# Attention probabilities scaled in place before the transpose, half blocks of two heads transposed together, half tile's values on 64 queries

## What is computed

```python
for e in range(4):
    q, k, v = x @ wq[e], x @ wk[e], x @ wv[e]
    scores = 64 ** -0.5 * (q @ k.T)                # then a causal mask
    a = exp(scores - max); a /= a.sum(-1) + 1e-9
    out += w_e * (a @ v @ wo[e])                   # w_e: gate of a token, 0 outside its best 2 experts
```

## Time and profile before

| | |
|---|---|
| median of 3 runs | 814.02 us (814.00 to 814.14) |
| the profiled execution's own time | 816.52 us |
| its span, first to last instruction | 814.4 us |
| granted TensorE clock, mean | 0.998 |
| TensorE busy | 798.5 us (98%) |
| VectorE busy | 489.7 us (60%) |
| ScalarE busy | 371.3 us (46%) |
| GpSimd busy | 186.3 us (23%) |

### The profile page before, as it was taken

The page is one execution under the profiler, slowest core; times in us unless marked ns, Lnnn a source line. Parts: engine busy times, 40 slices in busy tenths (PEclk is TensorE's granted clock), DMA queues, the critical chain, the costliest instruction groups (busy, mean ns, idle before and its releaser), DMA issues. The chain is left out here.

```text
span 814.4 us, 16834 instructions
## 1 busy us (share of the span) xinstructions
PE 798.5 (98%) x6605; PEld 720.0 (88%) x6605; DVE 489.7 (60%) x1293; ACT 371.3 (46%) x845; POOL 186.3 (23%) x239
## 2 busy tenths in 40 slices
PE   6999999999999999999999999999999999999998
PEld 5888989989899898989889898998989989898896
DVE  3878654675447855487444865468554675547740
ACT  2767423663345533556134752356323653355521
POOL 1641332013310233002330123301331013300220
PEclk9999999999999999999999999999999999999999
DMA  9956023030231205040050401404023000100001
GB/s 258 255 129 164 2 45 86 11 109 1 52 73 51 68 1 117 15 118 1 1 111 14 119 1 37 94 2 118 1 50 75 2 2 1 59 14 2 1 2 64
DMA packets 117405, 47.28 MB, mean 58 GB/s; under 512 B 94352, under 2 KB 110736, under 8 KB 117328
## 3 DMA queue, kind: packets, MB, share of 16 engines
q1 hardware_dynamic: 117328, 46.21, 22.6%
HBM read 35.19 MB, written 9.44 MB: 55 GB/s over the span
## 5 line engine op out<-in xcount | busy, mean ns | idle before, releaser
L1070 PE MATMUL w<-wsgT_s,big 128*128 128x288 f32 x768 | 107.6, 296 | 0.0
L1070 PE MATMUL t<-big,wqk_s 128*128 128x288 f32 x768 | 106.0, 296 | 1.0 <-DVE wsgT_s L950 0.9
L1070 PEld LDWEIGHTS w<-wsgT_s,big 128*128 128x128 f32 x768 | 104.0, 189 | 0.0
L1070 PEld LDWEIGHTS t<-big,wqk_s 128*128 128x128 f32 x768 | 102.5, 188 | 1.6 <-DVE wsgT_s L950 1.1
L1070 PE MATMUL w<-wout_s,big 128*128 128x512 f32 x396 | 99.1, 399 | 0.0
L610 POOL TENSOR_TENSOR yT<-squares,yT 128x256 fp32r<-128x256 f32 (+1 forms) x32 | 22.4, 699 | 316.8 <-ACT yT L740 316.8
L844 DVE CUSTOM_DVE_ANT_0 w<-w,causal 128x64 f32<-128x64 f32 (+4 forms) x160 | 75.3, 515 | 24.2 <-PE w L1101 23.1
L1070 PEld LDWEIGHTS w<-wout_s,big 128*128 128x128 f32 x396 | 72.9, 188 | 17.2 <-DVE big L887 1.6
L754 ACT ACTIVATE big<-work 128x576 fp32r<-128x576 f32 x32 | 21.9, 686 | 113.5 <-POOL work L633 94.3
L1070 PE MATMUL t<-w_s,yT 128*128 128x512 f32 x240 | 63.3, 404 | 0.0
L956 DVE TENSOR_REDUCE ss<-squares 128x8 f32<-128x512 f32 (+1 forms) x40 | 25.2, 630 | 62.6 <-ACT squares L690 62.5
(11 more groups left out here) (140 smaller groups left out, 1439.3 us busy)
## 6 DMA issues: line engine op xcount, KB each, us to landing
kin<-in_k_dram SPq DMA_DIRECT2D x8, 1024.0 KB, 6.2
vin<-in_v_dram SPq DMA_DIRECT2D x8, 1024.0 KB, 9.2
out_dram<-work SPq DMA_DIRECT2D x32, 256.0 KB, 2.1
qin<-in_q_dram SPq DMA_DIRECT2D x112, 72.0 KB, 2.4
staged_win<-in_moe_w_in_dram SPq DMA_DIRECT2D x4, 512.0 KB, 5.4
vin<-in_moe_w_sg_dram SPq DMA_DIRECT2D x4, 288.0 KB, 3.9
kin<-in_k_dram SPq DMA_DIRECT2D x8, 128.0 KB, 2.9
vin<-in_v_dram SPq DMA_DIRECT2D x8, 128.0 KB, 7.0
```

Source lines behind the costliest of these rows:

```text
L1070: last = nc.tensor.matmul(o, stationary(hs, c), mv(hm, c), start=c == of[0] and p == 0, stop=c == of[-1] and p == len(PASSES) - 1)
```

## The change

The gate and the inverse row sum are multiplied into a [128, 1] factor, and the probabilities themselves are multiplied by it in place before they are transposed: for the even n of a tile by ScalarE, for the odd n by VectorE. The padding columns of `probs` are thus free, and the layout is turned around: the keys of e = 0 are stored in reversed block order and end where those of e = 1 begin, so that the half block of 64 keys of e = 0 and that of e = 1 lie side by side and form one block of 128. A tile has 4t + 2 blocks in place of 4t + 4. The value tile of the first keys is arranged to match. `y_mul` goes; ScalarE and VectorE take the high and low parts of y from PSUM, and GpSimd has no part in it. Tile 0's weighted values are computed for its 64 real queries only.

```diff
-    T_UNITS = {t: [4] * (t + 1) if t < NT - 1 else [8, 8, 4] for t in range(NT)}
+    T_UNITS = {t: [4] * t + [2] if t < NT - 1 else [8, 8, 2] for t in range(NT)}
+    SCALE_GROUPS = [(0, 1), (2, 3), (4,), (5,), (6,), (7,), (8, 9)]
...
-        return [("pv", 2 * t), ("pv", 2 * t + 1), ("y_mul", t), ("yhi", t)]
+        return [("pv", 2 * t), ("pv", 2 * t + 1), ("yhi", t)]
...
-            plan += [("ranks", 0), ("g_exp", 0), ("weights", 0), ("qk", (0, 1)), ("scale", 0), ("qk", (EP, 1)), ("scale", 1),
+            plan += [("ranks", 0), ("g_exp", 0), ("weights", 0), ("qk", (0, 1)), ("scale", 0), ("scale", 1), ("qk", (EP, 1)),
                      ("qk", (1, 1))]
...
-        plan += [("scale", 2)] + values(0) if last else values(0) + [("scale", 2)] + KV
-        plan += [("s", 6), ("s", 7), ("T", 2), ("exp", 6)] + copies(2, 0) + [("exp", 7)] + copies(2, 1, 2) + [("scale", 3)] + values(1)
+        plan += [("scale", 2), ("scale", 3)] + values(0) + ([] if last else KV)
+        plan += [("s", 6), ("s", 7), ("T", 2), ("exp", 6)] + copies(2, 0) + [("exp", 7), ("scale", 4)] + copies(2, 1, 2) + [("scale", 5)] + values(1)
...
-    MLP = [("h", 0), ("weights", 1), ("scale", NT - 1), ("h", 1), ("gelu", 0), ("gelu", 1)] + values(3)
+    MLP = [("h", 0), ("weights", 1), ("scale", 6), ("h", 1), ("gelu", 0), ("gelu", 1)] + values(3)
...
+        def qk_bounds(m, h):
+            return (0, 320, S)[h:h + 2] if m == EP else (0, HALF, S)[h:h + 2]
+        def qk_pieces(m, h):
+            lo, hi = qk_bounds(m, h)
+            if m != EP:
+                return [(0, hi - lo, PAD + lo)]
+            return [(max(0, k0 - lo), k0 + w - lo, SP - k0 - w) for k0, w in [(0, PAD)] + [(PAD + P * b, P) for b in range(4)]
+                    if lo <= k0 < hi]
...
-                        nc.scalar.activation(vals[PAD:P, j, :], src(U)[PAD:P, 0:VW], ACT.Copy).then_inc(v_half, 1)
+                        x = src(U)
+                        nc.scalar.activation(vals[0:PAD, 0, 0:2 * HD], x[0:PAD, 0:2 * HD], ACT.Copy)
+                        nc.scalar.activation(vals[PAD:P, 0, 2 * HD:VW], x[PAD:P, 2 * HD:VW], ACT.Copy).then_inc(v_half, 1)
...
+                    elif kind == "scale":
+                        n = SCALE_GROUPS[j][0]
+                        if n % 2 == 0:
+                            act.wait_ge(scl_ready, count(part, len(SCALE_GROUPS), j + 1))
+                            for a in range(2):
+                                nc.scalar.activation(probs_of(n, a), probs_of(n, a), ACT.Copy,
+                                                     scale=row_inv[:, n, a:a + 1]).then_inc(scaled["act"], 1)
...
-                    nc.vector.tensor_tensor(
-                        probs[t % 2][:, :, :, 0:PAD].rearrange("p e a n -> p (e a) n"),
-                        invs.rearrange("p e (a d) -> p (e a) d", d=1).to_broadcast([P, E, PAD]),
-                        gate[:, t, :].rearrange("p (f d) -> p f d", d=1).to_broadcast([P, E, PAD]),
-                        ALU.mult).then_inc(row_scaled, 1)
+                    nc.vector.tensor_tensor(invs, invs, gates, ALU.mult).then_inc(scl_ready, 1)
+                    n = ns[-1]
+                    if n % 2 == 1:
+                        dve.wait_ge(scl_ready, count(part, len(SCALE_GROUPS), g + 1))
+                        for a in range(2):
+                            nc.vector.tensor_scalar(probs_of(n, a), probs_of(n, a), row_inv[:, n, a:a + 1], None,
+                                                    ALU.mult).then_inc(scaled["dve"], 1)
...
-                def y_scaled(t):
...
                 def y_low(t):
+                    o = PAD if t == 0 and part % 2 else 0
+                    x = ps[u.slot(part, ("y", t))][:, 0:2 * P].rearrange("p (e n) -> p e n", e=EP)
                     dve.wait_ge(yT_hi, count(part, NT, t + 1))
+                    give(nc.vector.tensor_tensor(yT[:, LO, :, P * t + o:P * (t + 1)], x[:, :, o:P],
+                                                 as_f32(yT[:, HI, :, P * t + o:P * (t + 1)]), ALU.subtract), ("y", t))
...
-                    pe.wait_ge(row_scaled, count(part, NT, t + 1))
-                    blocks = [(e, a, b) for e in range(EP) for a in range(2) for b in range(t + 1)]
+                    blocks = [(0, a, b) for a in range(2) for b in range(1, t + 1)] + [(None, a, 0) for a in range(2)]
+                    blocks += [(1, a, b) for a in range(2) for b in range(1, t + 1)]
...
+                            if (i, r) == (0, 0):
+                                wait_scaled(2 * t)
+                            if (e, a) == (None, 0):
+                                wait_scaled(2 * t + 1)
...
+                    real = PAD if t == 0 else 0
...
-                            last = nc.tensor.matmul(x[HD * a:HD * (a + 1), P * e:P * (e + 1)], vals[:, b, w:w + HD],
-                                                    turned(t, e, a, b), start=b == 0, stop=b == t,
+                            last = nc.tensor.matmul(x[HD * a:HD * (a + 1), P * e + real:P * (e + 1)], vals[:, b, w:w + HD],
+                                                    turned(t, e, a, b)[:, real:P], start=b == 0, stop=b == t,
                                                     skip_group_check=True)
```

More of the change, by code:

```diff
@@ L276, in moe_chain @@
         x_tile = [work[:, 512 * r:512 * (r + 1)] for r in range(2)]
-        sq_tile = sb("squares", [P, 512], F32)[:, :]
-        y_t = [sq_tile[:, 2 * P * r:2 * P * (r + 1)] for r in range(2)]
-        probs = [probs_0, staged[:, :].rearrange("p (e a n) -> p e a n", e=EP, a=2)]
+        sq_tile = staged[:, 0:512]
+        probs = [x.rearrange("p (a n) -> p a n", a=2) for x in (probs_0[:, :], staged[:, :])]
         pT = [work, qT_uT[:, :, :].rearrange("p c n -> p (c n)")]
@@ L702, in body @@
                         m, h = j
-                        nc.scalar.activation(big2[:, HI, m, PAD + HALF * h:PAD + HALF * (h + 1)], src(U)[:, 0:HALF],
-                                             ACT.Copy, scale=HD ** -0.5 if m < EP else 1.0).then_inc(qk_hi, 1)
+                        x = src(U)
+                        for lo, hi, o in qk_pieces(m, h):
+                            last = nc.scalar.activation(big2[:, HI, m, o:o + hi - lo], x[:, lo:hi],
+                                                        ACT.Copy, scale=HD ** -0.5 if m < EP else 1.0)
+                        last.then_inc(qk_hi, 1)
                     elif kind == "g_exp":
@@ L843, in maximum, with scale_rows @@
                     x = ps[slot][:, o:o + K]
-                    nc.vector.tensor_tensor_reduce(x, x, causal[:, SP - K:SP], -1.0, -MASKED, ALU.add, ALU.min,
+                    t = n // 2
+                    m0 = SP - P if t > 0 and n % 2 == 0 else SP - K
+                    nc.vector.tensor_tensor_reduce(x, x, causal[:, m0:m0 + K], -1.0, -MASKED, ALU.add, ALU.min,
                                                    neg_max[:, n, a:a + 1]).then_inc(max_ready, 1)
-                def scale_rows(t):
-                    for n in (2 * t, 2 * t + 1):
+                def scale_rows(g):
+                    ns = SCALE_GROUPS[g]
+                    for n in ns:
@@ L974, in body @@
                         if part == 0:
-                            nc.vector.memset(vals[0:PAD, 0, :], 0.0)
-                        give(nc.vector.tensor_tensor(vals[PAD:P, 0, :], ps[u.slot(part, U)][0:PAD, 0:VW], vals[PAD:P, 0, :],
+                            nc.vector.memset(vals[PAD:P, 0, 0:2 * HD], 0.0)
+                            nc.vector.memset(vals[0:PAD, 0, 2 * HD:VW], 0.0)
+                        x = ps[u.slot(part, U)]
+                        nc.vector.tensor_tensor(vals[0:PAD, 0, 0:2 * HD], x[PAD:P, 0:2 * HD], vals[0:PAD, 0, 0:2 * HD], ALU.add)
+                        give(nc.vector.tensor_tensor(vals[PAD:P, 0, 2 * HD:VW], x[0:PAD, 2 * HD:VW], vals[PAD:P, 0, 2 * HD:VW],
                                                      ALU.add), U)
@@ L983, in body @@
                         m, h = j
-                        cols = slice(PAD + HALF * h, PAD + HALF * (h + 1))
                         dve.wait_ge(qk_hi, count(part, 8, QK_NTH[j] + 1))
-                        give(nc.vector.scalar_tensor_tensor(
-                            out=big2[:, LO, m, cols], in0=ps[u.slot(part, U)][:, 0:HALF],
-                            scalar=HD ** -0.5 if m < EP else 1.0, in1=as_f32(big2[:, HI, m, cols]),
-                            op0=ALU.mult, op1=ALU.subtract), U)
+                        for lo, hi, o in qk_pieces(m, h):
+                            last = nc.vector.scalar_tensor_tensor(
+                                out=big2[:, LO, m, o:o + hi - lo], in0=ps[u.slot(part, U)][:, lo:hi],
+                                scalar=HD ** -0.5 if m < EP else 1.0, in1=as_f32(big2[:, HI, m, o:o + hi - lo]),
+                                op0=ALU.mult, op1=ALU.subtract)
+                        give(last, U)
                     elif kind == "s":
@@ L1091, in scores @@
                     V, slot, o, K = scores_at(n, 0)
```

(8 more changed lines are left out.)

94 lines of the change are left out of this document (38 added, 56 removed).

## The result

The changed kernel took 817.19 us (median of 7 runs, 815.24 to 821.24) against 814.12 us for the kernel before (7 runs, 814.00 to 814.68): ratio 1.0037, 95% interval 1.0021 to 1.0052. Measured once more beside later experiments it took 820.66 us (6 runs) against 815.94: 1.0051 (1.0032 to 1.0070). So it is slower, by 0.2 to 0.7%. The time lies inside the forecast range (808 to 819), but the forecast took no change for the likeliest (814.5) and measured is 3.1 us more. The forecast kept 817 to 821 for another cause, dearer scalings, which did not come true: that the number lies inside the range is in part luck.

What follows compares the result with a forecast made beforehand. TensorE bounds the kernel, with the ScalarE/VectorE softmax chain close behind, taking back its 1.34 us a batch. 8 x 0.1 + 8 x 0.05 - 0.3 = +0.9, taken as +0.5 on 814.02: 814.5 us, range 808 to 819.

Steps and rivals of the forecast that it cites:

- dearer scalings: Rival: ScalarE's scaling of the last two pairs and everything queued behind it take longer, 817 to 821 us; chance 0.26.
- Steps 1 to 5: Fifth batch's softmax chain: first maxima of tiles 2, 3, 4 at 449.65, 454.2, 460.0, last pair's at 463.86.
- step 3: Tile 3's exponentials end at 458.05; TensorE arrives 0.9 us earlier for tile 4's scores and waits 0.1 to 0.2 us.
- Step 6: After tile 4's exponentials: ScalarE scalings, table load, gelus, y's high part to 471.25; VectorE's copy of tile 4 ends 472.85.
- Step 7: Tile 4's weighted values start at 472.9, before 472.81: chain +0.1 us a batch where TensorE alone gives -1.34.
- The drain behind a table load: Ahead of the first gelu: the skill's rule of about 1.38 us on top, 11 us more in all; chance 0.01.
- The fall of the clock at the new wait: Rival: half clock behind the wait of about 1 us near tile 4's values, each batch: 13 us, 827; chance 0.04.
- The last batch: No k.v product fills in; the 2.04 us wait and half clock stay, two transposes less: -0.3 us.
- The step that failed: Scaling tiles 0 and 1 ahead of the second key copy: up to 0.2 us a batch without cover, counted as 0.
- that cover: Gaps hiding the key and value copies before tile 1's transposes; the early scalings eat about 0.6 us of them.
- the factor 8: Per-batch terms read in the fifth batch, taken for all eight: 8 x 0.1 + 8 x 0.05 - 0.3.
- The clock rival: Clock falling at the new wait near tile 4's values, once a batch: 13 us more, 827 us; chance 0.04.

Runs made afterwards that it cites:

- e9: Changed kernel, in the first batch alone the scalings of tiles 0 and 1 moved behind the second key copy and `wsgR`: 815.90 us, 0.9996 of the kernel before.
- e10: The changed kernel itself, unaltered, measured again on the same chip as e9: 820.66 us, 1.0051 of the kernel before.
- e2: Changed kernel with y's high part of tile 3 issued behind tile 4's three copies, in all batches: 812.70 us, 0.9966 of the kernel before.
- e5: Changed kernel with both scalings of head pair 8 (tile 4) moved from ScalarE to VectorE: 812.32 us, 0.9955 of the kernel before.
- e7: Changed kernel with tile 0's weighted values on all 128 queries again: 816.0 us in one execution, ordinary periods 99.05 to 99.10 and 95.02 to 95.05.
- e8: e2 with tile 0's weighted values on all 128 queries again: one execution, ordinary periods 98.31, 94.25, 94.26 us; no total given.
- e6: e2 with the first batch's scalings of tiles 0 and 1 moved behind the second key copy and `wsgR`: 809.40 us, 0.9926 of the kernel before.

## Why the prediction was right or wrong

**Steps 1 to 5: right.** On the fifth batch of the changed kernel, less the 2.21 us by which it begins later, the first maximum of tile 2 starts at 449.67 (forecast 449.65), of tile 3 at 454.03 (454.2), of tile 4 at 459.62 (460.0), and of the last pair at 463.61 (463.86). The 0.4 us too many at tile 4 are roundings upward, as the forecast suspected. TensorE's side of step 3 was wrong: it arrives at tile 4's scores 0.48 us earlier than before, not 0.9, and does not wait there; the 0.31 us stand one product earlier, at the fifth value product.

**Step 6: right.** Scaling ends at 468.27 (468.55), y's high part at 470.94 (471.25), the copy at 472.54 (472.85). The first gelu starts 3.5 us behind the last exponential, 2.2 more than before, where at least 1.3 more was forecast. The prices, by the groups of the changed kernel:

```profile
L766 ACT ACTIVATE probs<-probs,row_inv 128x576 f32<-128x576 f32 x16 | 11.5, 769 | 6.0 <-DVE row_inv L887 6.0
L766 ACT ACTIVATE probs<-probs,row_inv 128x64 f32<-128x64 f32 x16 | 4.7, 340 | 14.7 <-DVE row_inv L887 14.7
...
L892 DVE TENSOR_SCALAR probs<-probs,row_inv 128x576 f32<-128x576 f32 x16 | 7.6, 518 | 0.3
L892 DVE TENSOR_SCALAR probs<-probs,row_inv 128x64 f32<-128x64 f32 x16 | 3.3, 252 | 0.3
```

ScalarE's 769 ns meet the 0.78 taken; the rival of a dearer scaling is out. VectorE's 518 ns are under the 0.6 taken, about halfway to the lower bound of 0.45: (518 - 252)/512 = 0.52 ns a column. The low parts of y, which subtract one tensor from another, with the first in PSUM:

```profile
L926 DVE TENSOR_TENSOR yT<-t,yT 128x256 fp32r<-128x256 f32 x36 | 15.3, 424 | 35.9 <-ACT yT L759 35.8
...
L926 DVE TENSOR_TENSOR yT<-t,yT 128x128 fp32r<-128x128 f32 x4 | 1.1, 284 | 0.1
```

That is (424 - 284)/128 = 1.09 ns a column, about twice as much. The Trainium skill, VectorE: DVE Perf Modes, section "Mode 2×_2P — use both read ports for one tensor", says that an instruction whose only tensor source lies in SBUF, as does its result, can read it through both ports, two elements a cycle, in fp32 too, and that one with a second tensor or with an operand in PSUM cannot. The trace agrees: 0.52 against 1.09 ns a column. The forecast had not used it. It changes nothing here, since VectorE's branch runs beside ScalarE's.

**Step 7: right in kind.** The values start at 472.63 on the clock of before (forecast 472.9; before 472.81). Of these 0.18 us before the old start only 0.04 a batch is left at the next batch (forecast +0.15); where between them the rest goes I have not followed. The wait is 0.66 us where 0.8 to 1.1 was forecast, since TensorE already spends 0.31 us at the fifth value product and had less to spend: it was spared 1.10 us a batch, not 1.34. The ten transposes were priced at 0.11 us each and give 0.89 in all. Kept (0.04) and waited (0.66 and 0.31) add up to 1.01 of these 1.10. TensorE's busy time is 790.7 us, where "about 788" was forecast; most of that comes from the same term.

**The drain behind a table load: did not come,** as the trace of before said. The load starts at 470.50 and takes 1.28, the gelu follows at 471.79. **The fall of the clock at the new wait** did not come either.

**The last batch: -0.3 was right,** by the runs that compare. Where the granted clock is 0.86 to 0.88 in 745 to 757 us (before, e9, e10) the last part takes 91.1, 90.6 and 90.7 us. In the changed kernel's first profile the clock held there, behind the same wait of 1.9 us, and the last part took 89.3. That 1.4 us is the clock, which falls there in some executions and not in others; the forecast's "the wait stays and so does the half clock" took one execution for a rule.

**The step that failed** is the one sentence "Scaling tiles 0 and 1 ahead of the second key copy eats about 0.6 us of that cover; without it up to 0.2 us a batch comes on the path (0 in the sum)", together with the factor 8. I read that cover in the fifth batch. The first batch runs another list, in which `wsgR` stands between the key copies, already with a wait of 0.9 us before the change: no cover at all. It measured +2.0 us by the wait and 0 to 2.7 more by the clock behind it, against 0. The clock rival was weighed for the new wait at tile 4 only, not for this one. With that batch repaired (e9) the time is 0.9996 (0.9984 to 1.0008) of the kernel before, where the forecast of 814.5 is 1.0006.

**Shown and not shown.** Shown: most of TensorE's gain is taken back at tile 4's copy (e2, e5); tile 0's cut is free in the changed kernel and in e2 (e7, e8); the loss is the first batch's (e9). Read from the traces only: that the fifth value product's wait is what makes that cut free. Not tried: giving the fifth value product another PSUM tile, which might free its 0.17 to 0.31 us. Open: what decides whether the clock falls behind one and the same wait.

**A better version.** e6, with the change kept, one entry moved in the later part of the list and two in the first batch's: 809.40 us, 0.7% below the kernel before and, by the two kernels' ratios to it, 1.1 to 1.2% below the changed one. Its six ordinary periods are 98.3 to 98.6 and 94.3. Of the 1.10 us a batch that TensorE was spared it keeps about 0.7.

## What to carry to other kernels

Where a change moves an entry in a list that all engines follow, read its cover in every variant of the list: the first and last batch have other neighbours, and a slip there is not averaged away. When an operation is put on an engine with an in-order queue, list what is queued behind it up to the next item that the bound engine waits for; here four items, and moving one of them behind the copy was worth 0.7 us a batch, though its own ScalarE instruction takes 0.39. A saving on the bound engine counts only up to the next handoff whose margin is thinner than the saving. And where an idle time sometimes brings a lower clock, compare executions whose clock held before a difference of medians is put down to the code.

## What was not expected of the hardware

The granted clock behind one and the same wait of 3.10 us was 1.00 in one execution and 0.79 or 0.70 in others, with 0 to 2.7 us lost; the same for the wait of 1.9 us in the last batch (1.00 or 0.86 to 0.88, 1.4 us). Behind the wait for the first batch's data it held in the kernel before (2.81 us) and fell in e10 (2.70 us, the product behind it 4.10 us in place of 2.55). Waits of 0.66 and 1.12 us brought no fall in any profile here. Much of the spread between executions of one kernel (815.2 to 821.2) goes with it: the changed kernel's two quickest of the first seven runs had a mean clock of 1.0, the slowest 0.994. Another part is the start: the first value product began between 40.5 and 43.7 us in the twelve profiles.
